# The first four scores of the next attention tile ahead of the second pair's transposes, and ACT's copies between exponentials

## The chip, the core and the metric

The kernel runs on one core of one Trainium2 chip. A core has five engines that run side by side, each through its own list of instructions in order, and wait for each other by semaphores: TensorE (PE, matmuls; its weight loads are shown apart as PEld), VectorE (DVE), ScalarE (ACT), GpSimd (POOL) and SyncE (SP, which here issues DMAs). Matmuls write to PSUM, eight banks of 512 float32 columns in 128 partitions; DVE and ACT read it. The metric is the device time of one execution in microseconds, the median of several.

## What is computed

Three stages, one after the other. The change touches only the first, attention with a window of 128 keys and 4 sink keys, over 4 batches, 8 heads, 768 positions, head size 64:

```python
scores = scale * np.matmul(q, k.transpose(0, 1, 3, 2))
keep = is_sink | in_window            # first 4 keys, or 0 <= rel < 128
scores = np.where(keep, scores, -1000000000.0)
a = np.exp(scores - np.max(scores, axis=-1, keepdims=True))
a = a / (np.sum(a, axis=-1, keepdims=True) + 1e-09)
attn = np.matmul(a, v)
```

Its rows (3072 tokens of 512) then go through a top-1 mixture of 8 experts (router logits, a gate, two matmuls with relu between, a residual) and through a dense layer with squared relu.

## The kernel before

**Tiles.** Attention is cut into 24 tiles of 128 queries, all 8 heads of a tile together, in 4 pairs. A tile sees two blocks of keys, its own and the one before (264 columns with the sinks), or only its own if it is a batch's first (132). A loop of 27 passes is written out on every engine; pass i works on several tiles at once: tile i's scores and exponentials, tile i-1's products, tile i-2's output, tile i-3's routing.

**Engines in a pass.** PE: `scores` (L732, two matmuls a head, one head in one of banks 0 to 3), `turn` (L760, transposes of a pair's probabilities into bank 4 for pairs 0 and 2, bank 5 for pairs 1 and 3), the transpose of the sinks' probabilities (L745, bank 7), `product` (L787, and L780 for the sinks, bank 6), `logits` (L811), `rows_back` (L798, transposes of the output into bank 5), `ranks` (L826, L827) and `logits_back` (L817). DVE: `maximum` (L1022, mask and maximum of a head out of its bank into `score`), between these the small steps of the routing of two other tiles, `take_output` (`xT_a`, L1132), `take_logits` (L1146), `normalise` (`x_row`, L1123, reads bank 5), `reciprocals` (L1113). ACT: `exps` (L573, a head's exponential and its sum), `turned` (L586, the copy of a turned pair out of its bank into `probT`; L583 for the sinks), the gate's exponential (L613). POOL splits the sinks' probabilities (L516, L518) and scatters rows. SP issues the loads of q, k and v.

**Order and waits.** The order on each engine is written out by hand. What ties it: a score waits until the maximum of four heads before has freed its bank; an exponential waits for its maximum; `turn(i, k)` waits for the two exponentials and for its bank: pair 0 for the copy of the tile before's pair 2, pair 1 for `normalise` (`s_x`), pair 2 for the copy of pair 0, and pair 3 for the copy of pair 1 (`s_turned`). A product waits for its pair's copy, and the first one for `take_output`. `normalise` waits for `rows_back`.

**Weights.** In passes 13 to 20 ACT also makes a chunk of the first expert's upper weight parts (`w_hi`, L306), behind its copies, and in passes 14 to 21 DVE makes a chunk of the lower parts (`w_lo`, L311), between `reciprocals` and the next tile's maxima. In passes 1, 5, 11 and 17 DVE also makes the lower parts of the sinks' values (`vs_part`, L1137).

Of the kernel before, what the change touches and what calls it, by code (L numbers as in the profile page):

```python
# [28 lines left out]
TILES = B * NT  # L29
# [41 lines left out]
def build(nc, n_sink, window, qT, kT, v, v_sink, w_route, weights, out):  # L71
# [10 lines left out]
    with ctx:  # L82
# [165 lines left out]
        def own_load(i):  # L248

            return i  # L250

        def before_load(i):

            return i - 1 if i < NT else i + 1
# [13 lines left out]
        def is_first(i):  # L268

            return ORDER[i][1] == 0  # L270

        def blocks(i):

            own = own_load(i) % RING
            return [own] if is_first(i) else sorted((own, before_load(i) % RING))
# [9 lines left out]
        def width(i):  # L285

            return KB * len(blocks(i))

        def step_flags(i):

            return i < TILES, 0 <= i - 1 < TILES, 0 <= i - 2 < TILES, 0 <= i - 3 < TILES
# [8 lines left out]
        def upper_chunk(u, slot, f):  # L300

            if isinstance(u, int) and u == 0:
                nc.scalar.wait_ge(s_w0[f], 16)
            else:
                nc.scalar.wait_ge(s_w[f], 16 * u)
            nc.scalar.activation(w_hi[slot][:, f, :], w_raw[:, f, :], ACT.Copy).then_inc(s_whi, 1)  # L306
# [250 lines left out]
        def _(eng):  # L557
# [5 lines left out]
            def exps(i, heads):  # L563

                for h in heads:
                    eng.wait_ge(s_max, H * i + h + 1)
                    if h == 0 and i >= 2:

                        eng.wait_ge(s_turn, ITEMS * (i - 1))

                        eng.wait_ge(s_eps, i - 1)
                        eng.wait_ge(s_psink, i - 1)
                    eng.activation(prob[:, i % 2, h, 0:width(i)], score[:, i % 2, h, 0:width(i)], ACT.Exp, bias=neg_max[:, i % 2, h:h + 1],  # L573
                                   scale=-1.0, accum_out=row_sum[:, i % 2, h:h + 1]).then_inc(s_exp, 1)

            def turned(i, k):

                eng.wait_ge(s_turn, ITEMS * i + k + 1)
                if i >= 1:

                    eng.wait_ge(s_pv, ITEMS * (i - 1) + k + 1)
                if k == SINK:
                    eng.activation(sinkT[:, :], route_ps[:, SINKS:SINKS + P], ACT.Copy).then_inc(s_turned, 1)  # L583
                else:
                    cols = 2 * P * len(blocks(i))
                    eng.activation(probT[:, k, 0:cols], turn_ps[k % 2][:, 0:cols], ACT.Copy).then_inc(s_turned, 1)  # L586

            def upper_sinks(b):
                eng.wait_ge(s_vs[b % 2], 16 * (b // 2 + 1))
                if b >= 2:  # L590

                    eng.wait_ge(s_pv, ITEMS * NT * (b - 1))
                eng.activation(vs_part[:, b % 2, :], vs_in[:, b % 2, :], ACT.Copy).then_inc(s_vshi, 1)

            for i in range(TILES + 3):
                a, bb, c, d = step_flags(i)
                if i == 1:
                    upper_sinks(0)
                if a:
                    exps(i, (0, 1))  # L600
                if bb:
                    turned(i - 1, 2)
                if a:
                    exps(i, (2, 3))
                if bb:
                    turned(i - 1, 3)
                    turned(i - 1, SINK)
                if d:

                    eng.wait_ge(s_top, i - 2)  # L610
                    if i >= 4:
                        eng.wait_ge(s_slot, i - 3)
                    eng.activation(expl[:, :], logit[:, 1:LOGITS], ACT.Exp, bias=neg_top[:, 0:1], scale=1.0,  # L613
                                   accum_out=expsum[:, 0:1]).then_inc(s_gate, 1)
                if a:
                    exps(i, (4, 5))
                    exps(i, (6, 7))
                    turned(i, 0)
                    turned(i, 1)
                if i >= TILES - UNIT - 3 and i < TILES - 3:  # L620
                    upper_chunk(0, 0, i - (TILES - UNIT - 3))
                if a and i % NT == NT - 2 and i // NT + 1 < B:
                    upper_sinks(i // NT + 1)
# [90 lines left out]
        def _(eng):  # L714
# [3 lines left out]
            def scores(i, heads):  # L718

                at = blocks(i)  # L720
                for h in heads:
                    n = H * i + h
                    if h == 0:
                        eng.wait_ge(s_q[i % 3], 16 * (i // 3 + 1))
                        for n_load in {own_load(i), own_load(i) if is_first(i) else before_load(i)}:
                            eng.wait_ge(s_k[n_load % RING], 16 * (n_load // RING + 1))
                    if n >= SCORE_BANKS:

                        eng.wait_ge(s_max, n - SCORE_BANKS + 1)
                    rows = slice(h % 2 * D, h % 2 * D + D)  # L730
                    keys = k_in[rows, at[0]:at[-1] + 1:max(at[-1] - at[0], 1), h // 2, :]
                    eng.matmul(score_ps[n % SCORE_BANKS][:, 0:width(i)], q_in[rows, i % 3, h // 2, :], keys, start=True, stop=True).then_inc(s_score, 1)  # L732

            def turn(i, k):

                to = turn_ps[k % 2]
                if i == 0 and k == 0:
                    eng.wait_ge(s_ident, 1)
                if k == SINK:

                    if i == 2:
                        eng.wait_ge(s_top, 1)
                    wait(eng, s_route, i - 2)
                    eng.wait_ge(s_psink, i + 1)
                    ins = eng.transpose(route_ps[:, SINKS:SINKS + P], prob_sink[:, :, :, :, :].bitcast(F32).rearrange("p v s h k -> p (v s h k)"), ident[:, :])  # L745
                else:
                    eng.wait_ge(s_exp, H * i + 2 * k + 2)

                    if k >= 2:
                        eng.wait_ge(s_turned, ITEMS * i + k - 1)  # L750
                    elif k == 0 and i >= 1:
                        eng.wait_ge(s_turned, ITEMS * i - 2)
                    elif k == 1 and i >= 2:
                        eng.wait_ge(s_x, i - 1)
                    elif k == 1 and i == 1:
                        eng.wait_ge(s_turned, ITEMS * i - 1)
                    u = 0
                    for half in range(2):
                        for at in range(len(blocks(i))):
                            ins = eng.transpose(to[:, u * P:(u + 1) * P], prob[:, i % 2, 2 * k + half, at * KB + NS:(at + 1) * KB], ident[:, :])  # L760
                            u += 1
                ins.then_inc(s_turn, 1)
# [38 lines left out]
            def logits(i):  # L801

                if i == 0:
                    eng.wait_ge(s_wr, 16)
                eng.wait_ge(s_xT, i + 1)

                eng.wait_ge(s_turned, ITEMS * min(i + 2, TILES))
                if i >= 1:
                    eng.wait_ge(s_top, i)
                for p in range(PAIRS):  # L810
                    ins = eng.matmul(route_ps[p * LG:(p + 1) * LG, LGT:LGT + P], w_r[:, p, :], xT_a[:, p, :], start=True, stop=True)  # L811
                ins.then_inc(s_lgT, 1)

            def logits_back(i):

                eng.wait_ge(s_lgturned, i + 1)
                eng.transpose(route_ps[:, 0:P], lgT[:, :], ident[:, :]).then_inc(s_logit, 1)  # L817
# [12 lines left out]
            for i in range(TILES + 3):  # L830
                a, bb, c, d = step_flags(i)
                if bb:
                    turn(i - 1, 2)
                    turn(i - 1, 3)
                    turn(i - 1, SINK)
                if a:
                    scores(i, (4, 5, 6, 7))
                if bb:
                    for k in range(PAIRS):
                        product(i - 1, k)  # L840
                if c:
                    logits(i - 2)
                    rows_back(i - 2)
                if a:
                    turn(i, 0)
                if d:
                    ranks(i - 3)
                if c:
                    logits_back(i - 2)
                if a:  # L850
                    turn(i, 1)
                if i + 1 < TILES:
                    scores(i + 1, (0, 1, 2, 3))
                if bb:
                    product(i - 1, SINK)

# [478 lines left out]
```

## Time and profile before

| | us |
|---|---|
| median of 3 runs | 1007.64 (1007.07 to 1007.76) |
| the profiled execution | 1006.6 |
| its span | 1005.0 |
| PE busy in the span | 960.8 (96%) |
| DVE, ACT busy | 444.9 (44%), 411.4 (41%) |
| attention stage | from the start to about 212 |

In the profile the attention stage is the first eight or nine of 40 slices, where DVE and ACT are busy for seven to eight tenths; from slice 10 on almost all of the time is PE's alone. Numbers in brackets behind a timeline row are the idle time of that engine before the row, and what ended it.

### The profile page before, as it was taken

What the parts mean: (1) busy time and instruction counts of PE and PEld (TensorE: products, weight loads), DVE (VectorE), ACT (ScalarE), POOL (GpSimd) and SP (SyncE); (2) the same over time, 40 slices, a digit from 0 to 9 for tenths busy, and PEclk for the clock granted to TensorE, in tenths of its full rate; (3) what the DMA queues carried; (4) which work ended last, traced back from release to release, by engine and by line L of the source; (5) the groups of instructions that cost most, each with busy time, mean ns of one, the idle gap of its engine ahead of it and who ended that gap; (6) DMA issues with size and microseconds to landing.
All of it is one profiled execution on the core that took longest, in us unless ns stands there. A gap on an engine that the chain in (4) does not pass through costs nothing.

```text
span 1005.0 us, 16412 instructions
## 1 busy us (share of the span) xinstructions
PE 960.8 (96%) x5360; PEld 771.1 (77%) x5361; DVE 444.9 (44%) x1371; ACT 411.4 (41%) x957; POOL 75.9 (8%) x130
## 2 busy tenths in 40 slices
PE   7999999839999999969999999999999999999998
PEld 6777777728888888858888888888888888888886
DVE  5777888754555555525323223322322232222223
ACT  7888889713555555523213112221221231222212
POOL 3111112210111111110000000000000000000000
PEclk9999999959999999989999999999999999999999
DMA  5556664466466666640002000200010020002001
GB/s 183 158 173 204 201 215 142 143 226 210 146 241 208 247 200 238 222 153 27 1 1 85 1 1 0 84 0 0 24 59 0 0 83 0 0 0 83 0 0 42
DMA packets 42016, 100.55 MB, mean 100 GB/s; under 512 B 6013, under 2 KB 6141, under 8 KB 41968
## 3 DMA queue, kind: packets, MB, share of 16 engines
q1 hardware_dynamic: 36096, 87.33, 25.9%
q0 software_dynamic: 4720, 10.69, 3.0%
q10 hardware_dynamic: 1152, 1.93, 0.5%
q8 instruction: 25, 0.41, 0.2%
q14 instruction: 23, 0.19, 0.1%
HBM read 79.05 MB, written 25.82 MB: 104 GB/s over the span
## 4 chain that ended last, share of the span: by engine, by line
PE 92%; DVE 4%; DMA 2%; issue 1%; ACT 0%; SPq 0%; DVEq 0%; POOLq 0%; ACTq 0%
PE bank L949 27%; PE bank L963 27%; PE bank L872 10%; PE bank L891 9%; PE bank L732 5%; PE bank L787 4%; PE bank L760 3%; DVE x_row L1123 2%; PE bank L798 1%; PE bank L880 1%; PE bank L780 1%; PE bank L931 1%; PE bank L811 1%; PE bank L864 1%; DMA x_c<-x_rows 0%
## 5 line engine op out<-in xcount | busy, mean ns | idle before, releaser
L1259 DVE TENSOR_TENSOR g<-relu_c 128x512 f32<-128x512 f32 x96 | 66.5, 692 | 364.2 <-ACT relu_c L678 364.1
L678 ACT ACTIVATE relu_c<-bank 128x512 f32<-128x512 f32 x96 | 57.4, 598 | 387.8 <-PE bank L949 387.8
L949 PE MATMUL bank<-x_hi,w_lo 128*128 128x512 f32 x384 | 152.3, 397 | 0.9 <-DVE x_lo L1252 0.9
L963 PE MATMUL bank<-w_hi,g_lo 128*128 128x512 f32 x384 | 153.1, 399 | 0.0
L949 PE MATMUL bank<-x_hi,w_hi 128*128 128x512 f32 x384 | 152.6, 397 | 0.0
L949 PE MATMUL bank<-x_lo,w_hi 128*128 128x512 f32 x384 | 152.4, 397 | 0.0
L963 PE MATMUL bank<-w_hi,g_hi 128*128 128x512 f32 x384 | 152.0, 396 | 0.0
L963 PE MATMUL bank<-w_lo,g_hi 128*128 128x512 f32 x384 | 151.9, 395 | 0.0
L311 DVE TENSOR_TENSOR w_lo<-w_raw,w_hi 128x1024 fp32r<-128x1024 f32 x80 | 94.6, 1216 | 10.5 <-ACT w_hi L306 10.4
L573 ACT ACTIVATE prob<-score,neg_max 128x264 f32<-128x264 f32 (+1 forms) x192 | 93.2, 491 | 10.0 <-DVE neg_max L1022 9.0
L949 PEld LDWEIGHTS bank<-x_hi,w_lo 128*128 128x128 f32 x384 | 72.5, 189 | 18.9 <-issue 1.2
L949 PEld LDWEIGHTS bank<-x_lo,w_hi 128*128 128x128 f32 x384 | 72.6, 189 | 17.9
L949 PEld LDWEIGHTS bank<-x_hi,w_hi 128*128 128x128 f32 x384 | 72.5, 189 | 17.4
L963 PEld LDWEIGHTS bank<-w_hi,g_hi 128*128 128x128 f32 x384 | 72.3, 188 | 17.5
L963 PEld LDWEIGHTS bank<-w_lo,g_hi 128*128 128x128 f32 x384 | 72.4, 189 | 16.9
L963 PEld LDWEIGHTS bank<-w_hi,g_lo 128*128 128x128 f32 x384 | 72.2, 188 | 16.8
L1022 DVE CUSTOM_DVE_ANT_0 score<-bank,masks 128x264 f32<-128x264 f32 (+1 forms) x192 | 74.3, 403 | 21.6 <-PE bank L732 17.7
L306 ACT ACTIVATE w_hi<-w_raw 128x1024 fp32r<-128x1024 f32 x80 | 80.1, 1048 | 7.9 <-issue 7.9
L1263 DVE TENSOR_TENSOR g_lo<-g,g_hi 128x512 fp32r<-128x512 f32 x96 | 65.8, 686 | 7.7 <-ACT g_hi L684 7.7
L732 PE MATMUL bank<-k_in,q_in 64*128 64x264 f32 (+1 forms) x384 | 60.4, 407 | 5.0 <-DMA k_in<-in_kT 4.8
L684 ACT ACTIVATE g_hi<-g 128x512 fp32r<-128x512 f32 x96 | 59.9, 624 | 9.9 <-PE bank L963 9.9
L586 ACT ACTIVATE probT<-bank 128x512 f32<-128x512 f32 (+1 forms) x96 | 52.7, 552 | 22.3 <-PE bank L760 22.3
(132 smaller groups left out, 1312.1 us busy)
## 6 DMA issues: line engine op xcount, KB each, us to landing
w_raw<-in_weights SPq DMA_DIRECT2D x80, 512.0 KB, 5.3
x_c<-x_rows SPq DMA_DIRECT2D x28, 256.0 KB, 3.4
k_in<-in_kT SPq DMA_DIRECT2D x24, 264.0 KB, 3.9
q_in<-in_qT SPq DMA_DIRECT2D x24, 256.0 KB, 3.4
v_in<-in_v SPq DMA_DIRECT2D x24, 256.0 KB, 3.8
x_rows<-x_row SPq DMA_DIRECT2D x24, 256.0 KB, 3.2
out<-w_raw SPq DMA_DIRECT2D x12, 512.0 KB, 2.9
x_raw<-routed SPq DMA_DIRECT2D x19, 260.0 KB, 3.2
```

What stands on the lines that cost most here:

```text
L306: nc.scalar.activation(w_hi[slot][:, f, :], w_raw[:, f, :], ACT.Copy).then_inc(s_whi, 1)
L311: eng.tensor_tensor(w_lo[slot][:, f, :], w_raw[:, f, :], w_hi[slot][:, f, :].bitcast(F32), ALU.subtract)\
L573: eng.activation(prob[:, i % 2, h, 0:width(i)], score[:, i % 2, h, 0:width(i)], ACT.Exp, bias=neg_max[:, i % 2, h:h + 1], scale=-1.0, accu ...
L684: eng.activation(g_hi[:, f % 2, :], g[:, f % 2, :], ACT.Copy).then_inc(s_cghi, 1)
L732: eng.matmul(score_ps[n % SCORE_BANKS][:, 0:width(i)], q_in[rows, i % 3, h // 2, :], keys, start=True, stop=True).then_inc(s_score, 1)
L872: ins = eng.matmul(h_ps[half][:, :], x[:, c, :], w[:, c, cols], start=(c == 0 and k == 0), stop=(c == DC - 1 and k == 2))
L891: ins = eng.matmul(y_ps[:, :], h[:, c // 4, at], w[:, DC + c // 2, cols], start=(c == 0 and k == 0), stop=(c == FC - 1 and k == 2))
L949: ins = eng.matmul(hc_ps[f % 2][:, :], w[f // UNIT][:, f % UNIT, wcols], x[:, c, :], start=(c == 0 and n == 0), stop=(c == DC - 1 and n == 2))
L963: ins = eng.matmul(yc_ps[s][:, :], gg[:, f % 2, s * P:(s + 1) * P], w[f // UNIT][:, f % UNIT, DM:CH], start=(f == 0 and n == 0), stop=(f = ...
L1022: eng.tensor_tensor_reduce(score[:, i % 2, h, 0:width(i)], score_ps[n % SCORE_BANKS][:, 0:width(i)], masks[:, mask_kind(i), 0:len(blocks(i ...
L1259: eng.tensor_tensor(g[:, f % 2, :], relu_c[:, f % 2, :], relu_c[:, f % 2, :], ALU.mult).then_inc(s_cg, 1)
L1263: eng.tensor_tensor(g_lo[:, f % 2, :], g[:, f % 2, :], g_hi[:, f % 2, :].bitcast(F32), ALU.subtract).then_inc(s_cglo, 1)
```

## The change

On PE, `scores(i + 1, (0, 1, 2, 3))` stands ahead of `turn(i, 1)` where it stood behind it. On ACT, the copy of pair 1 leaves the end of pass i and goes into pass i+1, behind exponentials 0 and 1 of that pass's tile; the copies of pairs 2 and 3 follow exponentials 2 and 3 one by one.

```diff
@@ ScalarE, the loop of passes
                 if a:
                     exps(i, (0, 1))
                 if bb:
+                    turned(i - 1, 1)
+                if a:
+                    exps(i, (2,))
+                if bb:
                     turned(i - 1, 2)
                 if a:
-                    exps(i, (2, 3))
+                    exps(i, (3,))
                 if bb:
                     turned(i - 1, 3)
                     turned(i - 1, SINK)
...
                     exps(i, (4, 5))
                     exps(i, (6, 7))
                     turned(i, 0)
-                    turned(i, 1)
@@ TensorE, the loop of passes
                 if c:
                     logits_back(i - 2)
+                if i + 1 < TILES:
+                    scores(i + 1, (0, 1, 2, 3))
                 if a:
                     turn(i, 1)
-                if i + 1 < TILES:
-                    scores(i + 1, (0, 1, 2, 3))
                 if bb:
                     product(i - 1, SINK)
```

PE before, from `turn(i, 0)` (first row) over the rank and logit steps to `turn(i, 1)` (fifth row), the next tile's scores, the sinks' product, and the transposes of pairs 2 and 3 of the next pass:

```order
L760 MATMUL bank<-ident,prob 128x128 x4
L826 MATMUL bank<-onehot,lower 128x8
L827 MATMUL bank<-onehot,ones 128x8
L817 MATMUL bank<-ident,lgT 128x128
L760 MATMUL bank<-ident,prob 128x128 x4
L732 MATMUL bank<-k_in,q_in 128x264 x4
L780 MATMUL bank<-sinkT,vs_part 128x128 x4
L760 MATMUL bank<-ident,prob 128x128 x8
```

The same place after (its lines are numbered 3 higher):

```order
L763 MATMUL bank<-ident,prob 128x128 x4
L829 MATMUL bank<-onehot,lower 128x8
L830 MATMUL bank<-onehot,ones 128x8
L820 MATMUL bank<-ident,lgT 128x128
L735 MATMUL bank<-k_in,q_in 128x264 x4
L763 MATMUL bank<-ident,prob 128x128 x4
L783 MATMUL bank<-sinkT,vs_part 128x128 x4
L763 MATMUL bank<-ident,prob 128x128 x8
```

The four scores have changed places with the four transposes of pair 1; nothing else moved on PE.

ACT before, from exponentials 4 to 7 of one pass over the copies of pairs 0 and 1 to the end of the sinks' copy of the next pass:

```order
L573 ACTIVATE prob,row_sum<-score,neg_max 128x264 x4
L586 ACTIVATE probT<-bank 128x512 x2
L573 ACTIVATE prob,row_sum<-score,neg_max 128x264 x2
L586 ACTIVATE probT<-bank 128x512
L573 ACTIVATE prob,row_sum<-score,neg_max 128x264 x2
L586 ACTIVATE probT<-bank 128x512
L583 ACTIVATE sinkT<-bank 128x128
```

The same place after:

```order
L573 ACTIVATE prob,row_sum<-score,neg_max 128x264 x4
L586 ACTIVATE probT<-bank 128x512
L573 ACTIVATE prob,row_sum<-score,neg_max 128x264 x2
L586 ACTIVATE probT<-bank 128x512
L573 ACTIVATE prob,row_sum<-score,neg_max 128x264
L586 ACTIVATE probT<-bank 128x512
L573 ACTIVATE prob,row_sum<-score,neg_max 128x264
L586 ACTIVATE probT<-bank 128x512
L583 ACTIVATE sinkT<-bank 128x128
```

Behind the four exponentials now stands one copy (pair 0), not two; pair 1's copy is the one behind exponentials 0 and 1, pair 2's behind exponential 2, pair 3's behind exponential 3.

## Rows read from the trace of the kernel before

**Rows 1.** The page: the chain that ended last, by engine.

```profile
PE 92%; DVE 4%; DMA 2%; issue 1%; ACT 0%; SPq 0%; DVEq 0%; POOLq 0%; ACTq 0%
```

**Rows 2.** The chain of waits, pass 9: start, length in us, work.

```profile
80.11 0.70 DVE x_row L1123
...
81.58 1.09 PE bank L732 x8
...
84.27 1.31 PE bank L732 x7
...
88.58 0.70 DVE x_row L1123
```

**Rows 3.** Timeline, a pass without weight work: start, length, engine, instruction.

```profile
63.19 0.69 DVE L1123 TENSOR_TENSOR x_row<-bank,recip 128x512 f32<-128x512 f32 x1 [0.32 <-PE bank L798]
...
63.41 0.14 PEld L817 LDWEIGHTS bank<-ident,lgT 128*128 128x128 f32 x1
...
63.58 0.60 ACT L586 ACTIVATE probT<-bank 128x512 f32<-128x512 f32 x1 [0.54 <-PE bank L760]
...
64.00 0.41 PEld L760 LDWEIGHTS bank<-ident,prob 128*128 128x128 f32 x4 [0.46 <-issue]
...
64.59 0.75 PEld L732 LDWEIGHTS bank<-k_in,q_in 64*128 64x128 f32 x8 [0.17 <-issue]
...
65.33 0.43 DVE L1022 CUSTOM_DVE_ANT_0 score<-bank,masks 128x264 f32<-128x264 f32 x1 [1.03 <-PE bank L732]
65.68 0.52 PEld L780 LDWEIGHTS bank<-sinkT,vs_part 128*128 128x128 f32 x4 [0.34 <-ACT probT L586]
...
65.81 0.52 ACT L573 ACTIVATE prob<-score,neg_max 128x264 f32<-128x264 f32 x1 [0.52 <-DVE neg_max L1022]
...
66.14 0.86 PEld L760 LDWEIGHTS bank<-ident,prob 128*128 128x128 f32 x8
...
66.49 0.52 ACT L573 ACTIVATE prob<-score,neg_max 128x264 f32<-128x264 f32 x1
...
67.00 0.58 ACT L586 ACTIVATE probT<-bank 128x512 f32<-128x512 f32 x1
...
67.28 0.97 PEld L732 LDWEIGHTS bank<-k_in,q_in 64*128 64x128 f32 x8 [0.17 <-issue]
...
68.62 1.75 PEld L787 LDWEIGHTS bank<-probT,v_in 128*64 128x64 f32 x32 [0.37 <-issue]
```

**Rows 4.** Timeline, pass 14, with weight work.

```profile
120.56 0.69 DVE L1123 TENSOR_TENSOR x_row<-bank,recip 128x512 f32<-128x512 f32 x1 [0.32 <-PE bank L798]
...
121.28 1.17 DVE L311 TENSOR_TENSOR w_lo<-w_raw,w_hi 128x1024 fp32r<-128x1024 f32 x1
...
122.56 1.05 ACT L306 ACTIVATE w_hi<-w_raw 128x1024 fp32r<-128x1024 f32 x1
...
122.72 0.42 DVE L1022 CUSTOM_DVE_ANT_0 score<-bank,masks 128x264 f32<-128x264 f32 x1
...
124.64 0.98 PEld L732 LDWEIGHTS bank<-k_in,q_in 64*128 64x128 f32 x8 [0.17 <-issue]
...
125.99 1.76 PEld L787 LDWEIGHTS bank<-probT,v_in 128*64 128x64 f32 x32 [0.37 <-issue]
```

**Rows 5.** Groups of instructions in the attention stage: the lower weight chunks.

```profile
L311 DVE TENSOR_TENSOR w_lo<-w_raw,w_hi 128x1024 fp32r<-128x1024 f32 x8 | 9.4, 1181 | 0.0
```

**Rows 6.** Timeline, single rows of the passes that differ.

```profile
14.95 1.06 ACT L586 ACTIVATE probT<-bank 128x512 f32<-128x512 f32 x2
...
17.04 0.75 PEld L732 LDWEIGHTS bank<-k_in,q_in 64*128 64x128 f32 x8 [0.17 <-issue]
...
93.27 1.97 PE L787 MATMUL bank<-probT,v_in 128*64 128x128 f32 x32 [0.20 <-DVE xT_a L1132]
...
97.10 0.69 DVE L1137 TENSOR_TENSOR vs_part<-vs_in,vs_part 64x512 fp32r<-64x512 f32 x1
...
151.15 0.29 PEld L732 LDWEIGHTS bank<-k_in,q_in 64*128 64x128 f32 x2 [0.60 <-DVE neg_max L1022]
```

## The prediction

> **What bounds the kernel now.** I read the page first: its chain of waits is PE for 92% of the span [rows 1], so only what delays PE counts. The change touches only the attention stage, which is a loop of 27 passes, most of them 8.47 us long (from one `x_row` to the next, 80.11 to 88.58 [rows 2]). So I went to the chain of waits inside one pass [rows 2], and from there to the timeline, to see what each engine has in hand beside the chain: one pass without the weight work [rows 3], one with it [rows 4]. The reader is to see three things. PE runs from the output transposes to the end of the next products without a break but for two places: the second pair's transposes (`turn(i, 1)`) wait for `x_row` (DVE, L1123), and the second four scores take 1.31 us where the first four take 1.09, since they wait for banks that DVE's maxima free [rows 2]. ACT waits as well, 0.54 us before a copy and 0.52 us before its first exponential [rows 3]; so before the change its copies of pairs 0 and 1 are done in time that ACT has to spare, long before PE asks for them.
>
> I count in each pass from the start of `x_row`, and call that zero.
>
> **What is removed.** The change puts the four scores of tile i+1 where PE now waits. The load for the last transpose before the wait ends at 63.41 + 0.14 = 63.55; scores that follow transposes start 0.17 us after them (64.59 [rows 3]), so at 63.72, or +0.53, and `turn(i, 1)` after them finds `x_row` long done (+0.69). Nothing is added in work: the same matmuls, copies and exponentials, and the same DMAs. Were nothing else late, PE would win the gap between 63.55 and 64.00, 0.45 us [rows 3], and 1.31 - 1.09 = 0.22 us in the second scores [rows 2]: 0.67 us a pass.
>
> **What is late next.** `turn(i-1, 3)` writes bank 5 and so waits until ACT has copied pair 1 of tile i-1. That copy moved on ACT from the end of pass i-1, before the exponentials of tile i, to behind exponentials 0 and 1 of tile i. It now hangs on a chain that starts with the moved scores: scores on PE, maximum 0 on DVE, exponential 0, exponential 1, the copy. Its lengths are in [rows 3]: first score to maximum 0, 65.33 - 64.59 = 0.74; maximum 0 to exponential 1, 66.49 - 65.33 = 1.16; exponential 1 to the copy behind it, 67.00 - 66.49 = 0.51; the copy itself 0.58; about 0.10 until PE goes on (an estimate: from the end of `x_row` at 63.88 to PE's load at 64.00 it is 0.12). Queued on PE behind that wait are the sink transpose, the second scores, all the products and the output transposes: everything.
>
> The Trainium skill's page "TensorE: Matmul & The Clock Gate" (Architectural detail) says that ACT's and DVE's queues are strictly first in, first out. It is this that would hold a ready copy behind an exponential that still waits for its maximum; were ACT free to take the copy first, the loss below would not be there.
>
> **A pass without weight work** [rows 3]. The copy ends at 0.53 + 0.74 + 1.16 + 0.51 + 0.58 = +3.52, PE resumes at +3.62. PE alone would be ready after scores 1.09, four transposes and the sinks' matmuls (64.00 to 64.59 less the gap of 0.17, then 65.68 to 66.14: 0.42 + 0.46) and four more transposes, 0.42: at +2.92. So it waits 0.70 there. Four transposes with the gap behind them take 0.59 (64.00 to 64.59) and the sink transpose 0.11, so the second scores start at +4.32, against 67.28 - 63.19 = +4.09 now. But now they are held by maxima, and then they are not (maximum 0 comes at +1.27, a full 0.87 earlier): they take 1.09. The products start at +5.41, against 68.62 - 63.19 = +5.43. From there the pass is what it was. The change in such a pass is -0.02 us, that is nothing: the wait for `x_row` has become a wait for the copy of pair 1.
>
> **A pass with weight work** [rows 4]. DVE makes a chunk of `w_lo` (1.18 us, eight times in this stage [rows 5]) ahead of its maxima, at 121.28, and reaches maximum 0 at 122.72, +2.16, whether the scores are there or not. Earlier scores gain nothing here. Before the change the copy of pair 1 was already done when this happened; now it waits for it: 2.16 + 1.16 + 0.51 + 0.58 = +4.41, PE resumes at +4.51, second scores at +5.21 (+4.08 before), products at +6.30, against 125.99 - 120.56 = +5.43. A loss of 0.87 us a pass. ACT's own chunk (122.56, 1.05 us) now follows the copy of pair 0 at about +0.9, ends near +2.0 and is hidden before exponential 0 (2.16 + 0.48 = +2.64). ACT's later work fits: behind the copy come three exponentials, two copies and small work, and the pass grows to about 9.3 us.
>
> **The other passes.** Two of the eight weight passes stand at a batch boundary, where PE waited for the maxima already (0.60 at 151.15 [rows 6]); their loss lies between 0 and 0.87, I take 0.5. In two passes without weight work (5 and 11) DVE makes the lower sinks (0.69, [rows 6]) ahead of maximum 0, which takes it past +1.27 by about 0.5: +0.5 each. In two passes (10 and 22) the next tile is half as wide and the products waited for `xT_a` on DVE (0.20 at 93.27 [rows 6]), which follows the maxima and comes earlier now: a gain between 0 and 0.5, I take -0.3 each. In the first two passes ACT is the late one (its two copies at 14.95 run without a wait, straight before exponential 0, [rows 6]), and the copy of pair 1 goes behind two exponentials; the second scores, at 17.04 now, come up to 1.1 us later. Between 0 and 1.1; I take +0.8, nearer the upper end since ACT has no idle time there.
>
> **Sum.** 6 x 0.87 = 5.2; 2 x 0.5 = 1.0; eight plain passes -0.2; sinks +1.0; narrow -0.6; start +0.8: +7.2 us. Behind the attention stage nothing changes, and the stage's end is on the chain, so all of it arrives. The profiled execution took 1006.6 us (span 1005.0), so it would take 1013.8; it lies 1.0 under the median of 1007.64, and from the median the forecast is 1014.8. Its own range: a plain pass can be off by 0.15 either way (1.2 over eight), a weight pass by the same, the rest by about 1: 1012 to 1017.5. SP's loads that wait for scores are released about half a microsecond earlier; nothing on the chain of the pass waits for them.
>
> **Rivals.**
> A. The gap is simply won. The Trainium skill's "Perfetto Trace Analysis" (Optimization Strategy) says to find the gaps on the most contended engine and make what they wait for start sooner; by that this change wins. As a mechanism here: the copy of pair 1 reaches PE before it is asked for, so all of some 19 passes win 0.45 us, and the 12 without weight work 0.22 more: 11 us, or 996. For it: the wait for `x_row` does go. Against it: the copy would have to end by +2.9, and the three durations on ACT alone, after the first possible maximum, take it to +3.5 [rows 3]. Chance 0.08.
> B. No change: the weight passes' loss is taken up by a wait further on, as the DVE chain at the stage's end or a transfer. For it: only eight passes lose. Against: PE is the chain in each pass, and no row shows slack behind it. 1007.6. Chance 0.10.
> C. A heavier loss: with the pass at 9.3 us ACT's later exponentials reach into the next copy of pair 0, and the delay feeds itself. By my count the last exponential of a weight pass ends near +8.8 and that copy is due at about +9.7, so 0.9 us are to spare; if they went, at 0.6 us a pass over eight passes, 1019.6. Chance 0.10.
> Forecast: 0.72. The three rivals and it make 1.
>
> **The numbers.** 1014.8, the likeliest. The range must leave out no more than 2 in 10: from 1009.5 to 1018.5 it holds my case and the near half of C. About 0.2%, 2 us, is what a measurement of this kernel can tell from no change. Faster: A, 0.08. Within it: B with a little of my own case, 0.10. Slower: 0.82.
>
> **What would show it.** In the changed kernel's profile PE's idle time before L763 is released by ACT's copy (or shown as issue) at the fourth pair's transposes, not by `x_row`; the first scores start near +0.5. In plain passes `x_row` recurs every 8.4 to 8.5 us; in the six weight passes every 9.3. The maxima of plain passes follow zero by 1.3 us instead of 2.1. I am wrong if weight passes stay under 8.8 us, or if plain ones fall under 8.2: then the copy is not what PE waits for, or ACT runs faster than its rows.

## The result and the profile after

The changed kernel is slower: 1015.62 us as the median of four runs (1012.97 to 1016.4) against 1007.36 (1006.53 to 1007.76) beside them, a ratio of 1.0078 with a 95% interval of 1.0057 to 1.0099. The forecast was 1014.8. The profiled execution took 1012.97 us, its span 1011.4; it is the fastest of the four, and what it shows adds up to 6.4 us of span.

The waits of the attention stage in the changed kernel (engine, line waited for; us in total, times, longest):

```profile
PEld bank L763 <- ACT prob L573: 25.7, 21, 3.0
DVE lgT L1149 <- PE bank L814: 21.4, 22, 1.4
PE bank L763 <- ACT probT L586: 21.3, 21, 2.8
...
ACT prob L573 <- DVE neg_max L1025: 16.4, 19, 2.0
```

Before, PE waited for `x_row` 22 times, 7.3 us in all; one such wait of 0.5 us is left, in the pass that has no scores to move. PE's transposes (L763) now wait 21.3 us for ACT's copy, once in each of 21 passes. Where, a pass without weight work shows (pass 8, the answer to [rows 3]; timeline: start, length, engine, instruction, idle before):

```profile
73.08 0.69 DVE L1126 TENSOR_TENSOR x_row<-bank,recip 128x512 f32<-128x512 f32 x1 [0.32 <-PE bank L801]
...
73.55 0.75 PEld L735 LDWEIGHTS bank<-k_in,q_in 64*128 64x128 f32 x8
...
74.30 0.43 DVE L1025 CUSTOM_DVE_ANT_0 score<-bank,masks 128x264 f32<-128x264 f32 x1
...
74.78 0.52 ACT L573 ACTIVATE prob<-score,neg_max 128x264 f32<-128x264 f32 x1 [0.71 <-DVE neg_max L1025]
...
75.46 0.52 ACT L573 ACTIVATE prob<-score,neg_max 128x264 f32<-128x264 f32 x1
...
75.98 0.57 ACT L586 ACTIVATE probT<-bank 128x512 f32<-128x512 f32 x1
...
76.66 0.42 PEld L763 LDWEIGHTS bank<-ident,prob 128*128 128x128 f32 x4 [0.74 <-ACT prob L573]
...
77.36 0.75 PEld L735 LDWEIGHTS bank<-k_in,q_in 64*128 64x128 f32 x8 [0.17 <-issue]
...
78.45 1.73 PEld L790 LDWEIGHTS bank<-probT,v_in 128*64 128x64 f32 x32 [0.34 <-issue]
...
81.46 0.69 DVE L1126 TENSOR_TENSOR x_row<-bank,recip 128x512 f32<-128x512 f32 x1 [0.32 <-PE bank L801]
```

Counted from `x_row`: first scores at +0.47, maximum 0 at +1.22, the copy of pair 1 from +2.90, PE on again at +3.58, second scores at +4.28, products at +5.37. The pass lasts 8.38 us where it lasted 8.47. A pass with weight work, pass 14 (the answer to [rows 4]):

```profile
121.65 0.69 DVE L1126 TENSOR_TENSOR x_row<-bank,recip 128x512 f32<-128x512 f32 x1 [0.32 <-PE bank L801]
...
122.12 0.75 PEld L735 LDWEIGHTS bank<-k_in,q_in 64*128 64x128 f32 x8
...
122.37 1.17 DVE L311 TENSOR_TENSOR w_lo<-w_raw,w_hi 128x1024 fp32r<-128x1024 f32 x1
122.53 1.05 ACT L306 ACTIVATE w_hi<-w_raw 128x1024 fp32r<-128x1024 f32 x1
...
123.81 0.42 DVE L1025 CUSTOM_DVE_ANT_0 score<-bank,masks 128x264 f32<-128x264 f32 x1
...
125.47 0.58 ACT L586 ACTIVATE probT<-bank 128x512 f32<-128x512 f32 x1
...
126.16 0.42 PEld L763 LDWEIGHTS bank<-ident,prob 128*128 128x128 f32 x4 [1.67 <-ACT prob L573]
...
127.95 1.73 PEld L790 LDWEIGHTS bank<-probT,v_in 128*64 128x64 f32 x32 [0.34 <-issue]
...
130.95 0.69 DVE L1126 TENSOR_TENSOR x_row<-bank,recip 128x512 f32<-128x512 f32 x1 [0.32 <-PE bank L801]
```

Maximum 0 still comes at +2.16, behind DVE's weight chunk, and the copy, PE's next transposes and the products follow it: +3.82, +4.51, +6.30. The pass lasts 9.30 us where it lasted 8.47.

The pass that was forecast worst is pass 17. From its `x_row` at 148.72 to the next at 159.22 it lasts 10.50 us, where it lasted 8.47. DVE makes the sinks' lower parts (149.55) and a weight chunk (150.27) there before maximum 0, which comes at 151.76, +3.04, as it did before. Before its last transposes PE sits idle for 3 us, and then its clock is down (windows of 1 us: busy us and counts of PE, PEld, DVE, ACT, POOL; granted clock; DMA share; GB/s):

```profile
153.89 0.20 PEld L763 LDWEIGHTS bank<-ident,prob 128*128 128x128 f32 x2 [2.99 <-ACT prob L573]
```

```profile
153.00:154.00 1.00, 0.07 (x1) 0.11 (x2) 0.81 (x8) 1.00 (x4) 0.00 (x0) 1.00 0.02 6
154.00:155.00 1.00, 1.00 (x5) 0.72 (x7) 0.98 (x4) 1.00 (x6) 0.45 (x1) 0.63 0.07 16
155.00:156.00 1.00, 1.00 (x7) 0.69 (x6) 0.20 (x1) 0.76 (x5) 0.55 (x1) 0.50 0.02 8
156.00:157.00 1.00, 1.00 (x8) 0.43 (x6) 1.00 (x8) 0.72 (x3) 0.00 (x0) 0.50 0.38 131
157.00:158.00 1.00, 1.00 (x16) 0.94 (x12) 0.65 (x5) 1.00 (x5) 0.00 (x0) 0.67 0.28 68
```

### The profile page after: what moved, and what is told of

It reads as the page before. It is cut to its first block, busy times and chain, and to the rows that moved or that the text cites. A ratio compares the mean times of both kernels' runs of the same rounds, so it can differ in the third digit from the quotient of the medians.

```text
span 1011.4 us, 16412 instructions
## 1 busy us (share of the span) xinstructions
PE 952.9 (94%) x5360; PEld 764.5 (76%) x5361; DVE 446.7 (44%) x1371; ACT 410.8 (41%) x957; POOL 75.0 (7%) x130
## 4 chain that ended last, share of the span: by engine, by line
PE 89%; DVE 4%; issue 3%; ACT 2%; DMA 1%; DVEq 0%; SPq 0%; POOLq 0%; ACTq 0%
PE bank L952 27%; PE bank L966 27%; PE bank L875 10%; PE bank L894 9%; PE bank L790 4%; PE bank L735 3%; PE bank L763 2%; PE bank L883 1%; PE bank L801 1%; ACT probT L586 1%; PE bank L934 1%; DVE score L1025 1%; ACT prob L573 1%; PE bank L814 1%; PE bank L867 1%
## 5 line engine op out<-in xcount | busy, mean ns | idle before, releaser
L952 PE MATMUL bank<-x_hi,w_lo 128*128 128x512 f32 x384 | 151.6, 395 | 0.9 <-DVE x_lo L1255 0.9
L952 PE MATMUL bank<-x_hi,w_hi 128*128 128x512 f32 x384 | 152.1, 396 | 0.0
L952 PE MATMUL bank<-x_lo,w_hi 128*128 128x512 f32 x384 | 151.9, 396 | 0.0
L952 PEld LDWEIGHTS bank<-x_hi,w_lo 128*128 128x128 f32 x384 | 72.1, 188 | 18.8 <-issue 1.2
L952 PEld LDWEIGHTS bank<-x_lo,w_hi 128*128 128x128 f32 x384 | 72.1, 188 | 17.8
L952 PEld LDWEIGHTS bank<-x_hi,w_hi 128*128 128x128 f32 x384 | 72.2, 188 | 17.3
L763 PE MATMUL bank<-ident,prob 128*128 128x128 f32 x352 | 57.1, 282 | 22.6 <-ACT probT L586 22.0
L763 PEld LDWEIGHTS bank<-ident,prob 128*128 128x128 f32 x352 | 38.2, 142 | 35.7 <-ACT prob L573 26.8
```

The lines of the kernel that those rows point to most:

```text
L952: ins = eng.matmul(hc_ps[f % 2][:, :], w[f // UNIT][:, f % UNIT, wcols], x[:, c, :], start=(c == 0 and n == 0), stop=(c == DC - 1 and n == 2))
```

## The experiments

Two theories stood against each other. Mine: the time goes to PE's wait for pair 1's copy, which hangs on the moved scores through DVE and ACT, and most of all where a weight chunk stands ahead of maximum 0. The rival: moving four scores ahead of `turn(i, 1)` is itself the loss. Each kernel below was timed beside the kernel before.

**The PE part alone.** ACT's order as it was:

```diff
                 if c:
                     logits_back(i - 2)
+                if i + 1 < TILES:
+                    scores(i + 1, (0, 1, 2, 3))
                 if a:
                     turn(i, 1)
-                if i + 1 < TILES:
-                    scores(i + 1, (0, 1, 2, 3))
```

> The scores go ahead of turn(i, 1) on PE as in the change; ACT keeps the order of the kernel before (copy of pair 1 at the end of pass i). My theory (what costs is that pair 1's copy stands behind two exponentials that hang on the moved scores): the copy starts when turn(i, 1) has ended, near +2.3, and ends near +2.9, just when PE asks for it. Plain passes fall from 8.47 to about 7.8 us, passes with a w_lo chunk stay at 8.4 to 8.5 (DVE's maxima and take_output hold the products there). In all 5 to 8 us under the kernel before: 1000 to 1003. Rival (moving the scores is itself the loss, since turn(i, 1) and all behind it come 1.1 us later): as slow as the changed kernel, 1013 to 1016.

Measured: 1003.06 us, ratio 0.9959 (0.9947 to 0.9972): faster. Most plain passes last 7.75 to 7.77 us, pass 4 lasts 8.06; pass 5, with the sinks, lasts 8.23, and the six weight passes away from a batch boundary 8.47 to 8.50. Scores ahead of the transposes are a gain. The rival falls.

**The ACT part alone.** PE's order as it was:

```diff
                 if a:
                     exps(i, (0, 1))
                 if bb:
+                    turned(i - 1, 1)
+                if a:
+                    exps(i, (2,))
+                if bb:
                     turned(i - 1, 2)
                 if a:
-                    exps(i, (2, 3))
+                    exps(i, (3,))
...
                     turned(i, 0)
-                    turned(i, 1)
```

> ACT's order as in the change; PE keeps the order of the kernel before (scores behind turn(i, 1)). My theory: the chain scores, maximum 0, exponentials 0 and 1, copy now starts at +1.40 and not +0.53, so plain passes take 0.85 us more than before, 9.3, and the passes with a w_lo chunk 9.3 as in the changed kernel: about 18 us over the kernel before, 1025 (1021 to 1029). Rival (the loss comes from the scores' move): about 1007, as the kernel before.

Measured: 1025.15 us, ratio 1.0196 (1.0162 to 1.0229). A plain pass, pass 7 of this kernel, begins at 69.37:

```profile
69.37 0.69 DVE L1126 TENSOR_TENSOR x_row<-bank,recip 128x512 f32<-128x512 f32 x1 [0.32 <-PE bank L801]
...
70.76 0.75 PEld L735 LDWEIGHTS bank<-k_in,q_in 64*128 64x128 f32 x8 [0.17 <-issue]
...
73.18 0.57 ACT L586 ACTIVATE probT<-bank 128x512 f32<-128x512 f32 x1
...
73.87 0.42 PEld L763 LDWEIGHTS bank<-ident,prob 128*128 128x128 f32 x4 [1.13 <-ACT prob L573]
...
78.66 0.69 DVE L1126 TENSOR_TENSOR x_row<-bank,recip 128x512 f32<-128x512 f32 x1 [0.32 <-PE bank L801]
```

It lasts 9.29 us, and the copy starts 2.42 us after the first score (73.18 - 70.76), as it does in the changed kernel (75.98 - 73.55 = 2.43). The whole loss is in ACT's order; the PE part gave back about half of it (1025.15 to 1015.62).

**The copy one place earlier.** The changed kernel, with the copy behind one exponential:

```diff
                 if a:
-                    exps(i, (0, 1))
+                    exps(i, (0,))
                 if bb:
                     turned(i - 1, 1)
                 if a:
-                    exps(i, (2,))
+                    exps(i, (1, 2))
```

> The changed kernel with pair 1's copy behind exponential 0 alone (before it was behind 0 and 1 in the changed kernel). My theory: the copy ends 0.68 us earlier in every pass (1.16 from maximum 0 to exponential 1, less 0.48 to exponential 0), so PE's wait in plain passes goes (+2.94 against +2.92 ready) and they take 7.75 to 7.85; passes with a w_lo chunk lose 0.68 of their 0.87 and take about 8.6. In all 3 to 6 us under the kernel before: 1001 to 1005. Rival (PE does not wait for that copy but for something else that came with the change): no more than 0.5 us under the changed kernel.

Measured: 1000.37 us, ratio 0.9939 (0.9922 to 0.9955), 15 us under the changed kernel (12.7 between the profiled executions) for one exponential that changed places with a copy, and slightly under the range I gave. Plain passes last 7.76 us, weight passes 8.62. Pass 17 still takes 9.83: PE waits 2.31 us in it, and the granted clock is 0.50 afterwards. In a plain pass the third and fourth pairs' transposes are one row of eight again, with no wait between them:

```profile
71.25 0.60 ACT L586 ACTIVATE probT<-bank 128x512 f32<-128x512 f32 x1
71.42 0.97 PEld L763 LDWEIGHTS bank<-ident,prob 128*128 128x128 f32 x8
```

**The weight chunk out of the way.** The changed kernel, with DVE's chunk moved ahead of `take_logits`, where DVE waits for PE (0.89 us):

```diff
+                if i >= TILES - UNIT - 2 and i < TILES - 2:
+                    lower_chunk(eng, 0, 0, i - (TILES - UNIT - 2))
                 if c:
                     take_logits(i - 2)
                     normalise(i - 2)
...
-                if i >= TILES - UNIT - 2 and i < TILES - 2:
-                    lower_chunk(eng, 0, 0, i - (TILES - UNIT - 2))
```

> The changed kernel with one edit on DVE: the w_lo chunk of a pass is made ahead of take_logits, where DVE sits idle for 0.9 us, and not ahead of the next tile's maxima. My theory (a chunk ahead of maximum 0 is what makes the eight passes slow): maximum 0 comes at +1.3 in these passes too, they fall from 9.3 to 8.4 us, and pass 17 from 10.5 to about 9: 7 to 9 us under the changed kernel, 1005 to 1008. Rival (ACT's own chunk, or the mere length of ACT's list in these passes): they stay above 9 us, 1013 to 1016.

Measured: 1009.18 us, ratio 1.0019 (1.0009 to 1.0030), 6.4 under the changed kernel, 1.2 over what I gave. Its weight passes last 8.37 us (one of them 8.45), to 0.01 what its plain ones do, with ACT's chunk still in them: DVE's chunk ahead of maximum 0 is the whole difference, and ACT's is hidden. Pass 17 takes 9.26 us (I gave about 9), with a granted clock of 0.50 in it after a wait of 1.85 us. The stage ends 6.9 us earlier than in the changed kernel (208.69 against 215.59), near what I gave, but the profiled executions differ by only 5.0. The rest went in the last stage: its first layer (L952) begins at 451.3 and ends at 991.3, 2.1 us longer than in the changed kernel (458.3 to 996.2), and it begins at a granted clock of 0.50 (windows of 2 us, columns as above):

```profile
450.00:452.00 2.00, 1.14 (x5) 0.67 (x4) 1.53 (x3) 2.00 (x5) 0.00 (x0) 0.50 0.27 66
452.00:454.00 2.00, 2.00 (x7) 1.51 (x5) 2.00 (x3) 0.84 (x1) 0.00 (x0) 0.50 0.95 331
```

**The sinks' lower parts out of the way.** The changed kernel, with `lower_sinks` ahead of `take_logits`:

```diff
+                if a and i % NT == NT - 1 and i // NT + 1 < B:
+                    lower_sinks(i // NT + 1)
                 if c:
                     take_logits(i - 2)
...
-                if a and i % NT == NT - 1 and i // NT + 1 < B:
-                    lower_sinks(i // NT + 1)
```

> The changed kernel with one edit on DVE: the lower sinks (0.69 us, passes 5, 11 and 17) are made ahead of take_logits and not ahead of the next tile's maxima; the w_lo chunks stay. In the changed kernel PE stood idle 3.0 us in pass 17 and its clock was granted 0.50 afterwards. If the idle time is what brought the clock down there, PE idles some 2.3 us now, the clock stays at 1.00 and pass 17 falls from 10.5 to about 8.9 (0.7 for the sinks, 0.9 for the clock); if the clock falls all the same, to 9.8. Passes 5 and 11 win 0.5 to 0.7 each. In all 2 to 3.5 us under the changed kernel. Rival (the sinks cost nothing there): within 0.5 us of it.

Measured: 1011.66 us (1008.67 to 1016.36), ratio 1.0045 (1.0021 to 1.0068), 4.0 under the changed kernel and so a little more than the 2 to 3.5 I gave. Pass 5 falls from 9.05 to 8.37, pass 11 by 0.88. Pass 17 falls to 9.57, nearer to the second of my two readings: the shorter wait did not keep the clock up.

```profile
151.47 0.24 PEld L763 LDWEIGHTS bank<-ident,prob 128*128 128x128 f32 x2 [2.11 <-ACT prob L573]
```

```profile
150.00:152.00 2.00, 0.50 (x3) 0.45 (x3) 1.81 (x15) 1.93 (x8) 0.00 (x0) 0.89 0.38 127
152.00:154.00 2.00, 2.00 (x10) 1.19 (x8) 1.03 (x6) 1.33 (x7) 1.00 (x1) 0.50 0.15 39
```

**Both causes taken away.** The copy behind exponential 0, and the chunk ahead of `take_logits` (both diffs above):

> Pair 1's copy behind exponential 0 alone, and the w_lo chunk ahead of take_logits: the two causes taken away together. My theory: in the passes with a chunk maximum 0 comes at +1.3, the copy ends at +2.9, PE no longer waits for it, and they fall from 8.6 to 8.05 to 8.3, where ACT's own work of some 8.0 us becomes the bound. About 3 us under the kernel with the copy moved alone: 996 to 999. Rival (ACT's work or take_logits, held up by the chunk, takes the place of the wait at once): 8.6 or more in these passes, 1000 or above.

Measured: 996.47 us, ratio 0.9887 (0.9862 to 0.9911). Weight passes last 7.76 to 7.81 us, under what I gave: I had counted some 8.0 us for ACT's work in them, and ACT is busy for 7.41 us of such a pass. PE is busy in all of it (pass 14 as one window, columns as above):

```profile
114.00:121.81 7.81, 7.81 (x87) 6.15 (x85) 7.33 (x39) 7.41 (x24) 1.55 (x3) 1.00 0.72 231
```

**The PE part alone with the chunk moved.** ACT's order of before:

> The PE part alone (ACT in the order of before), with the w_lo chunk ahead of take_logits. The passes with a chunk were 8.49 us in the PE part alone. If DVE's late maxima held them, they fall to about 8.1; but ACT now has copy 1, its own chunk of 0.94 and the exponentials in a row from +2.3 on, so that pair 3's copy ends near +6.8, 0.6 after its product asks for it: then they stay at 8.4. I expect the second: 0 to 1.5 us under the PE part alone, 1001 to 1003.

Measured: 1000.53 us, ratio 0.9928 (0.9907 to 0.9948), slightly under the range I gave. Five of the six weight passes stay at 8.49 to 8.50 us. With maxima out of the way their products wait for ACT's copy (engine, line waited for; us in total, times, longest, over five passes):

```profile
PEld bank L787 <- ACT probT L586: 3.6, 5, 0.8
```

The passes with one chunk alone say the same. Pass 13, with ACT's chunk and none of DVE's, takes 8.50 us in the PE part alone and 8.49 here; pass 21, with DVE's and none of ACT's, falls from 8.47 to 7.76. So in these passes it does matter that the copy of pair 1 leaves the place ahead of ACT's weight chunk; the change was right to move it, and moved it one exponential too far.

**All three.** The copy behind exponential 0, chunk and sinks ahead of `take_logits`:

> Both edits and the lower sinks ahead of take_logits too. Passes 5 and 11 fall to 7.8; in pass 17 take_logits is held up by 1.9 us of DVE work and gives part of it back. 1 to 1.5 us under the kernel with both edits: 995 to 998. Rival (the hold-up of take_logits in pass 17 costs more than is won): as the kernel with both edits or above it.

Measured: 993.8 us, ratio 0.9860 (0.9844 to 0.9877), the fastest of all, 1.4% under the kernel before, and under the range I gave. Its plain and weight passes are alike (7.75 and 7.81 us); pass 17 takes 7.33. Of the waits of PE for the copy of pair 1 only one of 1.0 us is left, in pass 16. Pass 15, with both chunks:

```profile
123.16 0.58 ACT L586 ACTIVATE probT<-bank 128x512 f32<-128x512 f32 x1
...
123.25 0.42 PEld L763 LDWEIGHTS bank<-ident,prob 128*128 128x128 f32 x4
...
123.86 0.42 PEld L763 LDWEIGHTS bank<-ident,prob 128*128 128x128 f32 x4 [0.18 <-issue]
```

## Why the prediction was right, and where it was off

The mechanism was right, and most terms came out in the trace as they were worked out. That the total lies within 1 us of the forecast is in part luck: pass 17 and the start cost 2.0 us more than I gave them, the other passes 1.0 less, the last stage gave 1.4 back, and the three executions without a trace took 1.9 to 3.4 us more than the profiled one.

- **What is removed**: shown. Scores start at +0.47 (forecast +0.53: the gap before them is 0.11 here and not 0.17), PE's wait for `x_row` is gone. The PE part alone, with the copy in time, wins 0.70 us in a plain pass, against 0.67 counted.
- **What is late next**: shown, by the ACT part alone and by the copy one place earlier. PE resumes at +3.58 (forecast +3.62).
- **Plain passes**: 8.36 to 8.38 us, so about -0.09 each, against -0.02. Of the 0.07 more, 0.04 is there when the products start (+5.37, forecast +5.41).
- **Weight passes**: +0.82 to +0.84 each in five passes and +0.75 in pass 15, against +0.87. Maximum 0 at +2.16, PE at +4.51 and products at +6.30 are the forecast's numbers.
- **Pass 16**: +0.54; I took 0.5. **Passes 10 and 22**: -0.35 and -0.38 (-0.3). **Pass 5**: +0.59, **pass 11**: +0.37 (0.5 each). **Start**: the first `x_row` comes at 22.42, before at 21.15: +1.27, against 0.8; it lies above the upper end of 1.1 that I gave. The second scores that stood at 17.04 start at 18.31.
- **Pass 17** is the mis-sized term: +2.03, where I took 0.5. I counted the sinks' lower parts in passes 5 and 11 and left them out here, though DVE makes them in this pass too. The waits alone give the 0.5: its second scores start at 154.51, and 1.09 us for them would bring the products to 155.60, +6.88, where they stood at +6.31 before. The scores took 2.06 us, and from the products to the next `x_row` it is 2.65 us, before 2.16. Those 1.5 us are a halved clock, which no term of mine held.
- **"All of it arrives"**: nearly. The last `x_row` of the stage is 8.2 us late (215.59, before 207.40), and the first matmul behind it 8.1. In the profiled executions 1.4 us come back in the last stage, which begins 7.8 us late and ends 6.4 late. The granted clock was 0.50 as its first layer began in the kernel before, and 0.99 in the changed one; the longest matmul of that layer took 763 ns before and 471 after. In the kernel with the chunk moved this stretch at 0.50 was there again, so nothing shows that the change brought the gain. Before, then after (windows of 2 us with the columns as above; then count, ns of the shortest, middle and longest matmul, first and last start):

```profile
450.00:452.00 2.00, 1.47 (x4) 1.21 (x5) 2.00 (x4) 2.00 (x4) 0.00 (x0) 0.50 0.43 143
...
L949 PE MATMUL bank<-x_hi,w_lo x384: 388/394/763, 450.5 to 989.9; 128*128 128x512 f32 x192
```

```profile
458.00:460.00 2.00, 1.69 (x7) 1.43 (x8) 2.00 (x5) 1.85 (x3) 0.00 (x0) 0.99 0.68 203
...
L952 PE MATMUL bank<-x_hi,w_lo x384: 392/394/471, 458.3 to 996.2; 128*128 128x512 f32 x192
```

The other three runs of the changed kernel took 1014.85 to 1016.4, where the 6.4 us of the profiled one lead to 1013; their mean granted clocks are lower (0.979 to 0.981, against 0.983). They have no trace, so in which stage they lost it is open.

Of the rivals, A (the gap is simply won) is false for the change as it stands. Its mechanism holds for the PE part alone, and better with the copy one place earlier, but at 4.0 and 6.7 us and not the 11 it was given, since the weight passes win nothing or lose. B is false: the stage ends 8.2 us late. C did not occur: in pass 14 the last exponential ends at 130.36 and the next copy of pair 0 starts at 131.33.

## What to carry to other kernels

When work is moved ahead to fill a wait, look for what was cheap because of where it stood: here a copy that an engine did in its spare time became, by standing behind two exponentials, the next thing that PE waited for. The place in an in-order list is to be worked out as a chain (scores, maximum, exponential, copy), and one instruction's place decided 15 us of the medians, 12.7 between the profiled executions. Work that belongs to nobody's deadline, as a weight chunk, goes where its engine waits for another, not ahead of what starts the next chain.

## What was not expected of the hardware

A wait of PE can cost more than its length. After 3.0 us of idle PE in pass 17 the granted clock was 0.50 (1.2 GHz) from 155 to 157, and it cost another 1.5 us. It did not fall in the weight passes with a wait of 1.67 us before the same transposes, as the window of pass 14 around it shows (columns as above):

```profile
126.00:131.00 5.00, 4.81 (x60) 3.90 (x61) 3.22 (x18) 4.44 (x18) 1.41 (x3) 1.00 0.50 155
```

The length of the wait alone does not set this apart. These are the waits of over 1.8 us before the last transposes, with the tile half as wide in every one of them:

| kernel | pass | PE's wait, us | wait one pass earlier, us | granted clock afterwards |
|---|---|---|---|---|
| changed | 11 | 1.85 | 0.59 | 1.00 |
| changed, chunk moved | 11 | 1.85 | 0.59 | 1.00 |
| changed, chunk moved | 17 | 1.85 | 1.41 | 0.50 |
| changed, sinks moved | 17 | 2.11 | 1.72 | 0.50 |
| ACT part alone | 17 | 2.23 | 1.19 | 1.00 |
| changed, copy behind exponential 0 | 17 | 2.31 | 1.18 | 0.50 |
| changed | 17 | 2.99 | 1.72 | 0.50 |

The third and the fifth row are these (the kernel with the chunk moved, then the ACT part alone):

```profile
150.83 0.20 PEld L763 LDWEIGHTS bank<-ident,prob 128*128 128x128 f32 x2 [1.85 <-ACT prob L573]
...
152.00:155.00 3.00, 3.00 (x30) 1.83 (x26) 2.94 (x13) 2.68 (x12) 0.73 (x2) 0.50 0.48 137
```

```profile
164.15 0.20 PEld L763 LDWEIGHTS bank<-ident,prob 128*128 128x128 f32 x2 [2.23 <-ACT prob L573]
...
164.00:168.00 4.00, 3.82 (x43) 2.92 (x44) 3.40 (x18) 4.00 (x18) 1.00 (x1) 1.00 0.38 106
```

In pass 23 PE waits 1.9 us for other work in all ten kernels. The clock fell behind it in three of them, the ACT part alone, both causes taken away and all three edits, where the pass took 7.12, 7.59 and 7.64 us; it stayed at 1.00 in the other seven, where it took 6.15 to 6.16. What decides it stays open.
